# A causal mixing layer and two MLPs on one core: a quarter of weights fetched earlier, lone products on whole columns, one row of a mix on another engine

## The reference

```
w   = softmax(weight_gen, over 7 taps)            # per token, per head (8 heads of 24 features)
mix[t] = sum over k of w[t, head, k] * x[t - 6 + k]   # causal, zero in front of a sequence
h1  = mix @ w_in   (192 x 2048);  y1 = max(0.01 h1, h1) @ w_out   (2048 x 192)
h2  = y1 @ w2_in   (192 x 2048);  out = elu(h2) @ w2_out          (2048 x 192)
```

## Time and profile before

| What | us |
|---|---|
| Runs of the kernel | 1135.84, 1135.91, 1136.16 |
| Profiled execution, its own time | 1135.39 |
| its span in the trace | 1133.5 |
| busy: TensorE products | 1122.2 (99%) |
| busy: TensorE weight loads | 922.2 |
| busy: ScalarE | 742.3 |
| busy: VectorE | 629.9 |
| busy: GpSimd | 388.5 |

### The profile page before, as it was taken

One profiled execution on the slowest core, in us unless ns is written; L12 is line 12 of the kernel. 1 busy time (PEld: TensorE's weight loads), 2 busy tenths in 40 slices (PEclk: granted clock), 3 DMA queues, 4 the chain that ended last, 5 costly groups with the idle time before them and its releaser, 6 DMA issues.

```text
span 1133.5 us, 22700 instructions
## 1 busy us (share of the span) xinstructions
PE 1122.2 (99%) x9804; PEld 922.2 (81%) x9804; DVE 629.9 (56%) x663; ACT 742.3 (65%) x832; POOL 388.5 (34%) x406
## 2 busy tenths in 40 slices
PE   8999999999999999999999999999999999999998
PEld 5778888888888888888888888888888888888887
DVE  7776646455463654636456464554645546364455
ACT  4577757567575765757667575675757657576676
POOL 4744440806216071350804408052170713500000
PEclk9999999999999999999999999999999999999999
DMA  6313021120202102021020211202021020110001
GB/s 193 94 63 96 1 82 29 40 71 15 82 15 82 29 29 82 1 82 29 29 82 1 82 29 32 80 14 83 15 77 34 29 82 2 43 29 29 15 1 57
DMA packets 44724, 55.46 MB, mean 49 GB/s; under 512 B 4116, under 2 KB 32914, under 8 KB 44624
## 3 DMA queue, kind: packets, MB, share of 16 engines
q1 hardware_dynamic: 44624, 54.01, 15.7%
HBM read 36.29 MB, written 17.69 MB: 48 GB/s over the span
## 4 chain that ended last, share of the span: by engine, by line
PE 96%; DVE 3%; ACT 0%; DMA 0%; issue 0%; SPq 0%; ACTq 0%; DVEq 0%
PE y_a L665 30%; PE hidden L560 30%; PE y_b L648 20%; PE hidden L564 10%; PE hidden L615 5%; DVE hid_lo L1275 1%; DVE up_b_lo L1129 0%; DVE up_a_lo L1119 0%; PE hidden L622 0%; DMA wk<-in_weight_gen_dram 0%; ACT hid_hi L1023 0%; DVE prod L1137 0%; DVE staged L1137 0%; DVE act L1137 0%; PE y_a L795 0%
## 5 line engine op out<-in xcount | busy, mean ns | idle before, releaser
L665 PE MATMUL y_a<-hid_hi,dn 64*128 64x512 f32 x2048 | 625.5, 386 | 0.0
L665 PEld LDWEIGHTS y_a<-hid_hi,dn 64*128 64x128 f32 x2048 | 375.7, 184 | 40.1
L648 PE MATMUL y_b<-hid_hi,dn 64*128 64x512 f32 x1024 | 395.4, 386 | 0.0
L648 PE MATMUL y_b<-hid_lo,dn 64*128 64x512 f32 x1024 | 395.3, 386 | 0.0
L665 PE MATMUL y_a<-hid_lo,dn 64*128 64x512 f32 x1024 | 394.4, 386 | 0.0
L560 PE MATMUL hidden<-in_a_hi,up_a_hi 64*128 64x512 f32 x1020 | 295.1, 388 | 3.0 <-DVE hid_lo L1275 2.2
L560 PE MATMUL hidden<-in_a_lo,up_a_hi 64*128 64x512 f32 x1020 | 294.4, 386 | 0.0
L560 PE MATMUL hidden<-in_a_hi,up_a_lo 64*128 64x512 f32 x1020 | 294.3, 386 | 0.0
L564 PE MATMUL hidden<-in_b,up_b_hi 64*128 64x512 f32 x1020 | 294.3, 386 | 0.0
L1275 DVE TENSOR_TENSOR hid_lo<-hidden,hid_hi 128x1024 fp32r<-128x1024 f32 x124 | 151.6, 1223 | 252.1 <-ACT hid_hi L1023 251.9
L1275 DVE TENSOR_TENSOR hid_lo<-act,hid_hi 128x1024 fp32r<-128x1024 f32 x131 | 165.5, 1264 | 192.6 <-ACT hid_hi L1023 192.6
(11 more groups left out here) (118 smaller groups left out, 1313.8 us busy)
## 6 DMA issues: line engine op xcount, KB each, us to landing
xw<-in_x_dram SPq DMA_DIRECT2D x14, 960.0 KB
raw_b<-squares_out SPq DMA_DIRECT2D x60, 96.0 KB, 2.2
out_dram<-staged SPq DMA_DIRECT2D x15, 384.0 KB, 2.6
squares_in<-prod SPq DMA_DIRECT2D x56, 96.0 KB, 2.0
squares_out<-ya SPq DMA_DIRECT2D x15, 256.0 KB, 2.0
raw_a<-squares_in SPq DMA_DIRECT2D x14, 256.0 KB, 2.8
raw_d<-in_moe_w_out_dram SPq DMA_DIRECT2D x8, 384.0 KB, 4.4
raw_a<-in_moe_w_in_dram SPq DMA_DIRECT2D x8, 256.0 KB, 3.8
```

The source lines that it names most:

```text
L648: return nc.tensor.matmul(y_b[d // ST % 2][:, :], dn[m][rows, f, P:2 * P], v[rows, s % HB, HALF[i]], start=start, stop=stop)
L665: return nc.tensor.matmul(y_a[bank][:, :], dn[m][rows, f, w:w + P], v[rows, s % HB, HALF[i]], start=start, stop=stop)
```

## The change

1. **A third quarter of raw up weights.** A new tile `raw_third` takes the 128-row part of quarter 2 of MLP 1, and `ya` the rest; the softmax scratch moves from `ya` to a tile of its own. The quarter is fetched right behind the first down part, where the second down part was, and is rounded and split before step 0; the first down part is rounded and split behind step 0. The second down part is fetched behind quarter 3.
2. **Order of MLP 2's weights.** `UP2_AT` and `DN2_AT` change: quarter 0 goes from step 7 to step 8, quarter 1 from 8 to 9, quarter 2 from 11 to 13, quarter 3 from 13 to 15, down part 1 from 15 to 16. In phase 2 TensorE waits for each quarter in front of the step that first reads it.
3. **Whole columns.** Steps 1, 2, 8 and 10 use the new `up_whole`: eight products of 128 rows and the pair of 64 rows, with no wait for `s_open` inside.
4. **Two products with zeros** (128 x 512, added to the sum of chunk 0) stand in front of the last term's products.
5. **Row 3 of chunk 1's mix on VectorE.** GpSimd mixes rows 0 and 1, then row 2 alone. VectorE mixes row 3 in 13 instructions of 128x192: eight behind `hid_lo` of step 4 and five behind `hid_lo` of step 5, ahead of the down split there. The mix is signalled as ready when both are done.

```diff
@@ tiles
+        raw_third = sb("raw_third", [P, F // 4], f32)
+        top_all = sb("top", [P, J * H * 4], f32)
-        top = ya[:, 0:J * H * 3].rearrange("p (a k) -> p a k", k=3)
+        top = top_all[:, 0:J * H * 3].rearrange("p (a k) -> p a k", k=3)
...
@@ order of the weights of MLP 2
-        UP2_AT = [(0, 7), (1, 0), (1, 3), (1, 5)]
-        DN2_AT = [(1, 6), (1, 7), (2, 3), (2, 4)]
+        UP2_AT = [(1, 0), (1, 1), (1, 5), (1, 7)]
+        DN2_AT = [(1, 6), (2, 0), (2, 3), (2, 4)]
@@ place and wait of each raw quarter
+        RAW_UP = {(0, 0): (0, 0), (0, 1): (1, 0), (0, 3): (0, 2), (1, 0): (1, 4), (1, 1): (0, 8), (1, 2): (1, 10), (1, 3): (0, 12)}
+        def raw_up(m, q):
+            if (m, q) == (0, 2):
+                return raw_third, ya
...
@@ SyncE
             load_down(0, 0)
-            load_down(0, 1)
+            load_up(0, 2)
             sp.wait_ge(s_termv, FIRST_READS)
...
-            load_up(0, 2)
             load_up(0, 3)
+            load_down(0, 1)
             load_down(0, 2)
@@ GpSimd, mixing
+                ends = (J // 2, J - 1 if c == 1 else J)
                 for n in (0, 1):
-                    mix_taps(pool, nc.gpsimd, n * J // 2, (n + 1) * J // 2, ...)
+                    mix_taps(pool, nc.gpsimd, n * J // 2, ends[n], ...)
                 pool.wait_ge(s_mul, 2 * MIX_STEPS * c)
+                if c == 1:
+                    pool.wait_ge(s_mulv, MIX_STEPS)
@@ TensorE
+            def up_whole(m, src, s):
+                def product(i, w, v, **flags):
+                    cols = slice((2 * s + i) * P, (2 * s + i + 1) * P)
+                    return nc.tensor.matmul(hidden[:, s % 2, HALF[i]], w[m][:, cols], v[src][:, :], **flags)
+                for i in (0, 1):
+                    product(i, up_a_hi, in_a_hi, start=True, stop=False)
+                    product(i, up_a_lo, in_a_hi, start=False, stop=False)
+                    product(i, up_a_hi, in_a_lo, start=False, stop=False)
+                    product(i, up_b_hi, in_b, start=False, stop=False)
+                low, high = up_pair(m, src, s, stop=True)
...
@@ sum_first_mix
+                    if end:
+                        for _ in range(2):
+                            nc.tensor.matmul(turn_a, zeros[:, 0:P], zeros[:, :], start=False, stop=False)
@@ phase, TensorE
-                    if known(ph) and ph == 2 and s == 0:
-                        pe.wait_ge(s_uplo, 4 * QUARTERS)
+                    if ph == 2 and s % 2 == 0:
+                        pe.wait_ge(s_uplo, 2 * QUARTERS + s + 2)
...
+                    if ph == 0 and s < LAG or ph == 1 and s in (0, 2):
+                        up_whole(m, input_of(m, c), s)
+                        continue
                     up(m, input_of(m, c), g, s, False)
-                    if ph == 0 and s < LAG or ph == 1 and s in (0, 2):
-                        up(m, input_of(m, c), g, s, True)
-                        continue
@@ ScalarE: first_step, phase, before step 0
-                round_up(0, 2)
+                round_down(0, 0)
...
+                    if g in (2, 4, 5):
+                        round_down(0, (2, 4, 5).index(g) + 1)
                     if g == 2:
                         round_up(0, 3)
-                    if g in (1, 4, 5):
-                        round_down(0, (1, 4, 5).index(g) + 1)
...
-            round_down(0, 0)
+            round_up(0, 2)
@@ VectorE: first_step, phase, before step 0
+            def mix_last_row(first, last):
+                if first == 1:
+                    dve.wait_ge(s_x, x_arrived(1))
+                    dve.wait_ge(s_soft1, 7)
+                    dve.wait_ge(s_mixt, 1)
+                mix_taps(dve, nc.vector, J - 1, J, s_mulv, 0, (prod, prod2), wk[1], first, last)
...
-                split_up(0, 2)
+                split_down(dve, nc.vector, 0, 0)
...
+                    if (ph, s) == (0, 4):
+                        mix_last_row(1, 4)
+                    if (ph, s) == (0, 5):
+                        mix_last_row(4, TAPS)
...
-            split_down(dve, nc.vector, 0, 0)
+            split_up(0, 2)
```

More of the change, by code:

```diff
@@ L298, in known @@
             return isinstance(c, int)
-        def raw_columns(q):
-            return slice(q % 2 * F // QUARTERS, (q % 2 + 1) * F // QUARTERS)
+        RAW_UP = {(0, 0): (0, 0), (0, 1): (1, 0), (0, 3): (0, 2), (1, 0): (1, 4), (1, 1): (0, 8), (1, 2): (1, 10), (1, 3): (0, 12)}
+        def raw_up(m, q):
+            if (m, q) == (0, 2):
+                return raw_third, ya
+            half = RAW_UP[m, q][0]
+            cols = slice(half * F // QUARTERS, (half + 1) * F // QUARTERS)
+            return raw_a[:, cols], raw_b[:, cols]
         def raw_tiles(n):
@@ L319, in last_columns, with mix_taps @@
             return ap.rearrange("f (q j t) -> f q j t", q=Q, j=J)
-        def mix_taps(eng, ops, j0, j1, done, before, terms, weights):
+        def mix_taps(eng, ops, j0, j1, done, before, terms, weights, first=1, last=TAPS):
             n = len(terms)
@@ L332, in product @@
                 ops.tensor_tensor(dst, src, w, ALU.mult).then_inc(done, 1)
-            product(0)
-            product(1)
-            for k in range(1, TAPS):
+            if first == 1:
+                product(0)
+                product(1)
+            for k in range(first, last):
                 if k + 1 < TAPS:
@@ L363, in load_up @@
                 w_in = moe2_w_in if m else moe_w_in
[L364 to L370, removed]
+                if (m, q) in RAW_UP and RAW_UP[m, q][1]:
+                    sp.wait_ge(s_uplo, RAW_UP[m, q][1])
+                cols, (a, b) = slice(q * F // QUARTERS, (q + 1) * F // QUARTERS), raw_up(m, q)
+                sp.dma_start(a[:, :], w_in[0:P, cols]).then_inc(s_rawa[q], 16)
+                sp.dma_start(b[0:D2, :], w_in[P:D, cols]).then_inc(s_rawb[q], 16)
+                sp.dma_start(b[D2:P, :], w_in[P:D, cols]).then_inc(s_rawb[q], 16)
             def load_down(m, n):
@@ L640, in up_first @@
                 low.then_inc(s_up1, 1)
+                high.then_inc(s_up, 1)
+            def up_whole(m, src, s):
[8 more added lines that the diff above has]
+                low, high = up_pair(m, src, s, stop=True)
+                low.then_inc(s_open, 1)
                 high.then_inc(s_up, 1)
@@ L1112, in _, with split_up, tiles @@
         def _(dve):
[L1113 to L1128, removed]
-                        last = nc.vector.tensor_tensor(lo, tiles(raw_b, raw_columns(q)), tiles(up_b_hi[m]).bitcast(f32), ALU.subtract)
-                    last.then_inc(s_uplo, 1)
+            def split_up(m, q):
+                cols, (a, b) = slice(q * F // QUARTERS, (q + 1) * F // QUARTERS), raw_up(m, q)
+                dve.wait_ge(s_uphi, 2 * (QUARTERS * m + q) + 1)
+                nc.vector.tensor_tensor(up_a_lo[m][:, cols], a[:, :], up_a_hi[m][:, cols].bitcast(f32), ALU.subtract).then_inc(s_uplo, 1)
+                dve.wait_ge(s_uphi, 2 * (QUARTERS * m + q) + 2)
+                for i in (0, 1):
+                    rows = slice(i * D2, (i + 1) * D2)
+                    def tiles(ap):
+                        return ap[rows, :].rearrange("p (t i n) -> p t i n", i=2, n=P)[:, :, i, :]
+                    lo = up_b_lo[m][rows, q * F // QUARTERS // 2:(q + 1) * F // QUARTERS // 2].rearrange("p (t n) -> p t n", n=P)
+                    last = nc.vector.tensor_tensor(lo, tiles(b), tiles(up_b_hi[m][:, cols]).bitcast(f32), ALU.subtract)
+                last.then_inc(s_uplo, 1)
             def first_mixing():
```

11 lines of the change are left out of this document (6 added, 5 removed).

## The result

| | median us | runs | lowest to highest |
|---|---|---|---|
| before | 1135.95 | 12 | 1135.29 to 1136.73 |
| after | 1138.64 | 12 | 1137.07 to 1139.43 |

The ratio is 1.0021 with a 95% interval of 1.0013 to 1.0029. The change costs 2.7 us, and the interval excludes no difference. The forecast of 1135.0 us was wrong in sign and 3.6 us too low, and the time lies outside its range. The profiled execution of after took 1138.11 us with a span of 1136.3.

A forecast was written before the change was run, and what follows sets the result against it. TensorE was taken to bound (busy 1122.2 of 1133.5 us), with VectorE beside GpSimd nearly as full in the first 84 us. Terms +1.6 - 0.8 - 1.56 - 0.13 = -0.9 us gave 1135.0 us, 8-in-10 range 1132.4 to 1137.0.

The forecast's parts named there:

- part 3: Row mixed by VectorE: step 7 waits twice, and the turn of chunk 1 comes at 53.7, 1.6 us later.
- part 4: Behind the turn of chunk 1: 0.8 us gained up to step 8, then 1.56 up to 79.26.
- The start: Zeros before chunk 0's last term fill a 1.85 us pause, the clock stays up, step 0 ends 1.8 us earlier.
- the 17.7 that I had named as a sign of being wrong: Start of step 0's products: later than 17.7 us would show the forecast wrong.
- The price of VectorE beside GpSimd: Row mix on VectorE: instructions with two SBUF operands take turns with GpSimd's, 0.62 us per row instruction.
- the place of both waits: TensorE at step 7: a 2.7 us wait for hid_lo, and one for a down split inside the step.
- no wait at step 14: Step 14: the second wait for hid_lo goes, since a contended up split moved away.
- from the turn to step 8: Chunk 1's turn to step 8 takes 3.35 us instead of 4.15, a gain of 0.8.
- (b): Row on VectorE: each instruction costs 1.0 us, 1.4 in the first two; 1139.9 us in all, chance 0.12.
- (a): Row on VectorE costs what it costs alone, step 7 starts on time; 1131.8 us, chance 0.20 with its half case.
- (c): Row on VectorE under shared bandwidth: 0.49 us per instruction, 1133.3 us in all, chance 0.13.
- (d): Start: zeros do not hold the clock, 0.5 to 1.0 us arrives, 1135.7 us; chance within the forecast's 0.55.

The follow-up runs named there:

- e5: The changed kernel plus unread filler products, ten ahead of step 7's first wait and eleven ahead of its second; 1136.67 us, ratio 1.0010.
- e7: The kernel before with only the new order of MLP 2's weights and the wait per quarter; 1133.74 us, ratio 0.9985.
- e10: Like e6 but without the two products with zeros; 1131.47 us, ratio 0.9966.
- e8: The kernel before with only the two products with zeros added; 1135.6 us, ratio 1.0003.
- e6: The changed kernel with VectorE's row instructions spread: four behind hid_lo 4, four behind step 5's down split, five behind hid_lo 6; 1131.44 us, ratio 0.9963.
- e12: The kernel before with the weight order of e7 and the row placed as in e6; 1132.44 us, ratio 0.9974.
- e9: The kernel before with only chunk 1's row on VectorE, eight and five instructions as in the change; 1138.83 us, ratio 1.0028.
- e1: The changed kernel, but GpSimd mixes all four rows of chunk 1 again; 1136.8 us, ratio 1.0009.
- e2: The changed kernel plus eleven unread 128x512 filler products ahead of step 7's second wait; 1137.65 us, ratio 1.0013.
- e3: The changed kernel with step 5's down split ahead of the five row instructions instead of behind them; 1134.2 us, ratio 0.9988.
- e4: The changed kernel with lone steps 1, 2, 8 and 10 in pairs of 64 rows again; 1138.12 us, ratio 1.0018.

## Why the prediction was wrong, step by step

**The failed step** is in part 3: "Behind it stand 14 slots of step 7 and ten of the reversed down part, 5.44 us". I had put two waits of TensorE into step 7, 2.7 us and a second whose length I did not even write down, and then priced the 24 slots behind them at full clock. They took 7.61 us (48.86 to 56.47). With the pauses filled but VectorE as late, the clock stays up and step 8 comes 1.9 us sooner (e5). The row that warned of it was among mine: behind a pause of 1.85 us the clock of the kernel before stands at 0.50. I used it for the start alone and not for the longer pauses that my own sum created. With the 1.9 us that it cost the forecast would have been near +1.0, 1136.9 us.

**The mis-sized term** is in part 4: "Step 8 lasts 2.54 us for nine slots, 2.04". It lasts 2.38 on whole columns, and step 10 2.39. The stop behind L616 goes, but stops at the changes between 128 and 64 rows take its place: at the pair of 64 rows (L627) and at the first product of 128 rows (L659). These are their lines on the weight loads in the table of waits of after:

```profile
PEld hidden L627 <- issue: 1.8, 5, 0.4
...
PEld hidden L659 <- issue: 1.2, 4, 0.4
```

For steps 8 and 10 that is 2 x 0.35 = 0.7 us, all of the gap in the third line of the table above. I had excluded a restart without a row for it. The 2.54 us were no measure of pairs either: in e7, where step 8 does not wait for `in_b`, it takes 2.40 in pairs.

**The start was 0.8 us late.** The zeros took 1.99 us as forecast (1.9) and the clock stayed up. But the products of step 0 began at 17.74 and not at 17.3, just behind the 17.7 that I had named as a sign of being wrong, and L627 ended at 20.36, not 19.55. One half of the delay is that TensorE reached the zeros some 0.7 us later than the rows of before let expect. Of that 0.4 us arrive at step 0. The first eight products of chunk 0's sum took nearly twice as long; the first row is from before, the second from after:

```profile
6.87 1.16 PE L789 MATMUL y_b<-ident,prod 128*128 128x128 f32 x8 [0.18 <-DVE prod L1137]
6.68 2.07 PE L819 MATMUL y_b<-ident,prod 128*128 128x128 f32 x8
```

TensorE's program is the same up to there, and the group differs from execution to execution: 1.16 us in e7, 1.32 in e10, 1.66 in e8, 1.82 in e6, 2.00 in e12, 2.07 in e9. The other half is step 0 itself, 2.62 us against 2.24, with a stop like those of steps 8 and 10. From there the sum holds: `hid_lo` 0 to the end of `hid_lo` 4 took 22.67 to 38.03, 15.36 us (forecast 15.4), and step 6 started at 38.19 (37.4). Half of the 0.8 is made good at the row, whose five last instructions end at 47.79 (47.4). The down split then takes 1.0 us and not 0.8, and the down part of step 7 starts at 48.86 and not at 48.2.

**The sum of the misses** at step 15 is 86.46 - 82.8 = 3.7 us: 0.7 for the later down part, 2.2 for the 24 slots (1.9 of it the clock), 0.2 behind the turn, 0.7 for whole columns.

**What held.** The price of VectorE beside GpSimd, by turns and not by size (0.64 us per row instruction, forecast 0.62); the place of both waits; GpSimd done at 47.65 (forecast 47.3) and no longer late, though it started at 22.92 and not at 22.1 to 22.3; no wait at step 14; from the turn to step 8 3.53 us (forecast 3.35); nothing lost or gained behind step 15. The Trainium skill, page "SBUF — State Buffer", section "Who interferes with whom", was the rule behind the first of these, and the trace of after agrees (0.64 us under GpSimd, 0.35 in e6 where GpSimd is done).

**The rivals.** None named the cause. (b) had the sign, but its mechanism, 1.0 us per row instruction, is excluded by 0.64. (a) and (c) are excluded by the same number. (d) did not come about: in after the clock is 1.00 from 14 to 20 us. What the start is worth is open in part: e8 shows that a faster start alone ends in later waits, and in e10 the time is the same without the zeros.

## What to carry to other kernels

Where a change makes TensorE wait, and waits as long have brought its clock down in the traces at hand, price the work behind the wait at half clock too; here two waits of 4.6 us together cost 1.9 more in what ran behind them. When a busy engine takes over work, put that work behind the result that the bounding engine needs next, and let its tail fall where the other engine is done: the same 13 instructions cost 1.6 us in one order (after against e1) and gained 5.3 in another (e6 against e1). A faster start was worth nothing here (e8) while the inputs of the next meeting points came no earlier.

## What the runs showed of the hardware

- The pause in front of the last term of chunk 0 does not always bring the clock down. Behind 1.85 us it fell in two executions (before, and e7, where it was 0.61 in 16 to 18 us). Behind 1.69 us in e10 it stayed at 1.00, as it did in e9 and e12, where the pause was only 0.73 and 0.93.
- The pauses of the other stages fall on the same two sides. Behind 1.85 us (e9 at 26.41), 1.89 to 1.93 (step 7 of e2, e3 and e4), 2.14 (e9) and 3.57 (e1) the clock went to 0.50. Behind 1.44 and 1.56 us (e8 at 26.43 and at the turn) and 1.54 (before at 36.34) it stayed at 1.00. No run varied the length alone, so that it is the length that decides is not shown.
- It fell at different moments behind the waits of step 7: in e2 at once behind the first (0.67 in 44 to 46), in after in 46 to 48, in e9 from 50 on. In after it came back at 53 us, some 7 us later, in e2 near 48.
- The eight products 128x128 at 6.7 to 6.9 us took from 1.16 to 2.07 us in different executions, with a granted clock of 1.00 in the rows of before and of after alike. The later they end, the shorter the pause before the last term: 1.85 us behind 1.16, 0.73 behind 2.07.
- Eleven products of 128x512 took 3.76 us where most of them ran at the lower level, and 2.79 at the upper.
- Eight products of 128 rows and a last pair of 64 rows take as long as nine pairs of 64 rows with a semaphore between them, 2.39 us (after and e4), though each of the two stops in other places.
